# Expert stage of a fused attention and MoE kernel: the second halves of the weight split divided between VectorE and GpSimd and moved to the end of a tile

## Chip, cores, metric

One core of a Trainium2 chip. The metric is device time in microseconds (us) of one execution. TensorE is called PE below, VectorE DVE, ScalarE ACT, GpSimd POOL and SyncE SP, as the profile names them.

## The reference, cut to what matters

Linear attention (8 batches, 8 heads, 576 rows, 64 columns) gives 4608 rows of 512. A gated product with four weight matrices follows, and then the stage that the change touches, a top-1 mixture of 8 experts:

```python
logits = x @ w_gate                       # 4608 x 8
expert_idx = np.argmax(logits, axis=1)
gate_w = probs[np.arange(N), expert_idx]  # softmax of the logits
for e in range(E):
    mask = expert_idx == e
    h = np.maximum(x[mask] @ w1[e], 0.0)  # 512 -> 1024
    out[mask] = gate_w[mask, None] * (h @ w2[e])  # 1024 -> 512
```

## The kernel before

**Precision.** All products are of float32 data in three passes (`split3`, L166): each operand is split into a high part, rounded to the type that PE multiplies (`fp32r`), and a low part, which is the operand less its high part; high by high, high by low and low by high are summed. Every operand of PE so costs a rounding copy (the high part) and a subtraction (the low part).

**Tiles.** The expert stage (from L849 on, in the blocks of `stage2`) works on tiles of 128 rows of one expert. A tile's row numbers stand in a table that the program makes from the counts, and so do the tile's expert and a planned chunk number (below). With the inputs used there are 40 tiles: 5, 4, 5, 1, 5, 5, 8 and 7 for the eight experts. Tiles 0 to 2 are written out, tiles 3 to 38 run in a loop on each engine (`tiles`, one iteration a `tile(g)` or `period(g)`), and the last is written out again.

**One tile on PE** (`tile`, in the PE block): the first product of tile g in two halves (24 matmuls), the transposition of the gathered rows of tile g+1 (4, L1669), and the second product of tile g-1 (24). PE waits in front of them for semaphores that stand for: the rows' low part (`xt_lo`), the rectified halves (`relu_done`), the turned h's low part (`ht_lo`), a result copied out (`y_sb`), and the weights' low part (`w_lo`).

**One tile on the other engines, before.** ACT: four rectifying pieces of the first half times two (8 ACTIVATEs, L1244), the rows' high part (L1200), the high parts of the weight chunks that the table gives this tile (`tile_chunks`, L809), the next gate (L1210), the turned h's high part (L1251). DVE: 8 pieces of the second half (L1451), with the rows' low part (L1428) after the third of them, then the turning of h in 32 by 32 blocks (STREAM_TRANSPOSE, L1461), the copy of the result (L1435), the turned h's low part (L1466). POOL (`period`): gather of tile g+2 by an indirect DMA (L1058, L1061), the low parts of this tile's weight chunks (L1104), scatter of tile g-1 (L1068, L1072).

**Weight chunks.** An expert's weights are 4 chunks of 128 x 2048 (1 MB): two of w1, two of w2. SP loads them into 4 slots (`ahead`), ACT writes the high part into a ring of 8 chunks, then POOL subtracts and writes the low part. SP loads chunk c into its slot when the low part of chunk c-4 is made. The table row CH says up to which chunk a tile goes: it is made on DVE by a chain of small operations (L1541 to L1569) from the tiles' experts, as early as the ring allows and no later than the products need. With these inputs the table of before gives 26 chunks to tiles: two chunks to each of tiles 12, 13 and 15, one to twenty others. Chunks 4 and 5 are written out before the loop.

**The first tiles.** POOL gathers the rows of tiles 1 and 2 (`first_gather`, L1040) when the gate of the tile before is taken over (`gate_set`). For tile 1, ACT copies the gate aside (`gnext`, L1204, which increments `gate_saved`) right after the rows' high part, and takes it over (L1210, `gate_set`) after the rectifying of tile 0.

The loop of chunks, as each engine that has a part in it runs it (L922 to L933):

```python
def tile_chunks(eng, g, body):
    first = table(m, eng, CH, g - 1, CPE, NCH)
    end = table(m, eng, CH, g, CPE, NCH)
    chunks(eng, first, end, body)
```

`table` (L823) is a load of a table entry into a register with a range check.

Of the kernel before, what the change touches and what calls it, by code (L numbers as in the profile page):

```python
# [29 lines left out]
ds = bass.ds  # L30
# [795 lines left out]
def stage2(nc, m, t):  # L826

    with ExitStack() as ctx:
# [25 lines left out]
        w_hi, w_lo = m["w_hi"], m["w_lo"]  # L854
        lg_mm, lg_shift, lg_exp = sem("s2_lg_mm"), sem("s2_lg_shift"), sem("s2_lg_exp")
# [90 lines left out]
        def _(sp):  # L946
# [69 lines left out]
        def _(pool):  # L1016
# [68 lines left out]
            for g in range(1, FIRST):  # L1085
                pool.wait_ge(gate_set, g)
# [36 lines left out]
            last1, last2 = last_of(pool, 1), last_of(pool, 2)  # L1123
            keep_gate(last)
            tile_chunks(pool, last1, weights)
            scatter(last2)
            tile_chunks(pool, last, weights)
# [5 lines left out]
        def _(act):  # L1133
# [93 lines left out]
            def h_high(g):  # L1227
                late = not isinstance(g, int)
                if late:
                    act.wait_ge(w_lo, NCH)  # L1230
                elif g > 0:
                    act.wait_ge(y_mm, g)
# [50 lines left out]
            tile_chunks(act, last, weights)  # L1283
# [3 lines left out]
        def _(dve):  # L1287
# [156 lines left out]
            def relu_moved(g):  # L1444
# [30 lines left out]
            dve.sem_inc(h_turned, 1)  # L1475
            turns(dve, turn)
# [58 lines left out]
            for h in range(2):  # L1535
# [5 lines left out]
            linked(dve.tensor_scalar(ch, ch, 1.0 / CPE, 1.0, ALU.mult, ALU.min), base)  # L1541
            linked(dve.scalar_tensor_tensor(ch, ch, 1.0, ex, ALU.add, ALU.add), base)

            linked(dve.scalar_tensor_tensor(ahead_of[:, 0:last_g], ex[:, 1:last_g + 1], 1.0 / CPE,
                                            ex[:, 2:last_g + 2], ALU.add, ALU.max), base)
            linked(dve.scalar_tensor_tensor(ahead_of[:, 0:last_g], ahead_of[:, 0:last_g], 2.0 / CPE,
                                            ex[:, 3:last_g + 3], ALU.add, ALU.max), base)
            linked(dve.tensor_tensor(ch[:, 0:last_g], ch[:, 0:last_g], ahead_of[:, 0:last_g], ALU.max), base)

            linked(dve.scalar_tensor_tensor(ahead_of[:, 1:last_g], ex[:, 0:last_g - 1], early_w2,  # L1550
                                            ex[:, 2:last_g + 1], ALU.add, ALU.min), base)
            linked(dve.scalar_tensor_tensor(ch[:, 1:last_g], ahead_of[:, 1:last_g], 2.0,
# [252 lines left out]
```

## Time and profile before

| | |
|---|---|
| median of 3 runs | 1511.0 us (1509.08, 1511.07, 1511.0) |
| profiled execution, its own time | 1509.39 us |
| its span in the profile | 1507.7 us |
| PE busy | 1473.6 us, 98% of the span |
| mean granted TensorE clock | 0.993 |
| expert stage | about 1036 to 1498 us of the span |

The span is what the trace covers; the own time of the execution is 1.7 us longer. The profile names a group of instructions by line, engine, operation and tiles (out<-in); most buffers lie in one tile called `arena`, the ring is `big`, the split rows and h are `xs`. PEq, ACTq and so on are an engine's sequencer, which runs register instructions.

### The profile page before, as it was taken

The page shows a single profiled execution, that of the slowest core. Times are in us where ns is not written, and L with a number is a line of the kernel's source. Part 1 is how long each engine was busy: PE and PEld are TensorE (multiplying, and loading weights), DVE is VectorE, ACT ScalarE, POOL GpSimd, SP SyncE. Part 2 cuts the span into 40 slices and gives each one's busy share as a digit, 9 for nine tenths or more (in the row PEclk, how much of TensorE's full clock was granted, in tenths as well). Part 3 has the DMA queues.
Part 4 walks back from the last instruction along what each step waited for, and adds up shares of the span by engine and source line. Part 5 has one row for each costly group of instructions (what it writes and reads, how often), then busy time and mean ns, then how long its engine had stood idle before and what let it go on. Part 6 is the DMA issues. An engine that isn't in the chain of part 4 may idle for free.

```text
span 1507.7 us, 28846 instructions
## 1 busy us (share of the span) xinstructions
PE 1473.6 (98%) x8070; PEld 1274.8 (85%) x8071; DVE 979.4 (65%) x1877; ACT 713.0 (47%) x1512; POOL 630.7 (42%) x681
## 2 busy tenths in 40 slices
PE   7999999999999999999999999999999899999997
PEld 6999999999978888888888888887888778888885
DVE  5688888888825374655637465535677777777663
ACT  5688788788812122121212212143566566656442
POOL 6676676676810021020202102021667776665221
PEclk9999999999999999999999999999999999999999
DMA  7354344344430202021120202134424433321110
GB/s 254 115 142 107 104 107 107 103 108 127 109 122 0 71 15 84 0 84 28 56 70 14 84 0 84 29 131 153 167 96 141 163 116 130 125 73 49 40 48 23
DMA packets 84601, 134.67 MB, mean 89 GB/s; under 512 B 50016, under 2 KB 50272, under 8 KB 80338
## 3 DMA queue, kind: packets, MB, share of 16 engines
q1 hardware_dynamic: 76978, 114.01, 25.2%
q0 software_dynamic: 7584, 20.17, 4.2%
q8 instruction: 21, 0.34, 0.1%
q14 instruction: 18, 0.15, 0.0%
HBM read 104.26 MB, written 30.94 MB: 90 GB/s over the span
## 4 chain that ended last, share of the span: by engine, by line
PE 67%; DVE 1%; DMA 1%; POOL 1%; issue 1%; ACT 1%; POOLq 0%; ACTq 0%; DVEq 0%
PE bank L166 65%; PE bank L1669 1%; POOL big L1104 1%; DVE xs L1466 1%; DMA arena<-rows_scratch,ids 1%; ACT arena L1244 0%; DMA out<-arena,ids 0%; DVE arena L1451 0%; PE bank L1600 0%; PE bank L1705 0%; PE bank L1619 0%; PE bank L1608 0%; ACT big L809 0%; PE bank L1594 0%; DVE xs L1428 0%
## 5 line engine op out<-in xcount | busy, mean ns | idle before, releaser
L166 PE MATMUL bank<-big,xs 128*128 (+1 forms) x2088 | 492.6, 395 | 14.7 <-DVE big L609 8.1
L166 PEld LDWEIGHTS bank<-big,xs 128*128 128x128 f32 x2088 | 391.7, 189 | 96.7 <-issue 15.8
L166 PE MATMUL bank<-xs,big 128*128 128x512 f32 x1728 | 397.4, 391 | 2.7 <-PEq L215 2.7
L166 PEld LDWEIGHTS bank<-xs,big 128*128 128x128 f32 x1728 | 324.7, 188 | 70.3 <-issue 2.9
L166 PE MATMUL bank<-big 128*128 128x512 f32 (+1 forms) x1632 | 325.8, 348 | 2.0 <-POOL big L305 1.4
L166 PEld LDWEIGHTS bank<-big 128*128 128x128 f32 (+1 forms) x1632 | 255.8, 165 | 36.2 <-POOL big L305 1.7
L1021 POOL TENSOR_TENSOR arena<-arena 128x512 f32<-128x512 f32 x32 | 39.8, 1255 | 440.5 <-DMA arena<-rec_scratch 440.2
L1397 DVE TENSOR_TENSOR arena<-arena,bank 128x512 f32<-128x512 f32 x72 | 49.4, 686 | 246.0 <-PE bank L166 246.0
L1157 ACT COPY arena<-bank 128x512 f32<-128x512 f32 x72 | 42.3, 587 | 306.9 <-PE bank L166 302.6
L1322 DVE CUSTOM_DVE_ANT_0 arena<-arena 128x512 f32<-128x512 f32 x256 | 159.5, 688 | 14.9 <-ACT arena L1177 14.7
L1451 DVE TENSOR_SCALAR arena<-bank,gate 32x256 f32<-32x256 f32 x288 | 138.9, 482 | 44.5 <-PE bank L166 40.1
L703 PE MATMUL bank<-arena 128*128 128x66 f32 (+1 forms) x1152 | 147.6, 269 | 0.0
L1244 ACT ACTIVATE arena<-bank,gate 32x256 f32<-32x256 f32 x288 | 134.6, 467 | 17.0 <-PE bank L166 13.9
L703 PEld LDWEIGHTS bank<-arena 128*128 128x128 f32 x1152 | 142.3, 191 | 0.2
L1104 POOL TENSOR_TENSOR big<-arena,big (+1 forms) x28 | 131.9, 4716 | 21.6 <-ACT big L809 10.3
L180 POOL TENSOR_TENSOR kqs<-kqraw,kqs 128x256 fp32r<-128x256 f32 (+1 forms) x160 | 130.1, 813 | 12.8
L507 ACT ACTIVATE arena<-arena 128x256 f32<-128x256 f32 (+1 forms) x320 | 110.3, 399 | 50.0 <-DVE arena L633 40.0
L166 PE MATMUL bank<-wphis,kqs 128*128 128x256 f32 x864 | 130.9, 291 | 0.3
L621 DVE TENSOR_REDUCE absmax<-bank 128x4 f32<-128x512 f32 (+1 forms) x160 | 100.7, 629 | 23.3 <-PE bank L166 22.6
L633 DVE TENSOR_TENSOR arena<-bank,absmax 128x512 f32<-128x512 f32 (+1 forms) x160 | 102.2, 639 | 18.4 <-ACT arena L507 0.5
L166 PEld LDWEIGHTS bank<-wphis,kqs 128*128 128x128 f32 x864 | 111.3, 189 | 1.7 <-DVE arena L633 1.2
L305 POOL TENSOR_TENSOR big<-qeraw,big 128x768 fp32r<-128x768 f32 x32 | 58.7, 1836 | 88.8 <-DMA kqraw<-kq 79.3
(175 smaller groups left out, 1395.0 us busy)
## 6 DMA issues: line engine op xcount, KB each, us to landing
arena<-we SPq DMA_DIRECT2D x32, 1024.0 KB, 4.8
kqraw<-kq SPq DMA_DIRECT2D x32, 576.0 KB, 3.8
rows_scratch<-arena SPq DMA_DIRECT2D x36, 256.5 KB
xT_scratch<-arena SPq DMA_DIRECT2D x32, 288.0 KB
arena<-v SPq DMA_DIRECT2D x64, 128.0 KB, 2.4
arena<-xT_scratch SPq DMA_DIRECT2D x8, 1024.0 KB, 5.4
arena<-rec_scratch SPq DMA_DIRECT2D x64, 128.0 KB, 3.8
arena<-w3T SPq DMA_DIRECT2D x8, 512.0 KB, 3.4
```

Of the source, the lines that this page charges most:

```text
L166: ins = nc.tensor.matmul(out, left[a], right[b], start=first and n == 0, stop=last and n == 2)
L180: pool.tensor_tensor(m["kqs"][:, 1, u, cols], m["kqraw"][:, u, cols], m["kqs"][:, 0, u, cols].bitcast(F32), ALU.subtract).then_inc(m["kq_l ...
L305: eng.tensor_tensor(qes[:, 1, :, cols], qeraw[:, :, cols], qes[:, 0, :, cols].bitcast(F32), ALU.subtract).then_inc(qlo_done[n], 1)
L507: last = act.activation(ke[:, rows[0]:rows[-1] + 1, s * P:(s + 1) * P], pm[:, rows[0]:rows[-1] + 1, 0], ACT.Exp, scale=1.0 - 2.0 * s)
L621: dve.tensor_reduce(absmax[:, bank, 0:n], proj_ps[bank][:, 0:2 * n * P].rearrange("p (t a f) -> p t a f", t=n, a=2), AX.X, ALU.max, apply_ ...
L633: dve.tensor_tensor(pm[:, rows[0]:rows[-1] + 1], proj_ps[bank][:, 0:2 * n * P].rearrange("p (t a f) -> p t a f", t=n, a=2), absmax[:, bank ...
L703: last = pe.matmul(kv_ps[:, s, cols[0]:cols[1]], ke[:, r, s * P:(s + 1) * P], v[:, u, slots[0]:slots[1]].rearrange("p t d -> p (t d)"), st ...
L1104: pool.tensor_tensor(ring[:, 1, ds(at, CW)], ahead[:, ds(slot, CW)], ring[:, 0, ds(at, CW)].bitcast(F32), ALU.subtract).then_inc(w_lo, 1)
L1244: last = act.activation(hq[a * Q:(a + 1) * Q, b * QF:(b + 1) * QF], h_ps[0][b * Q:(b + 1) * Q, a * QF:(a + 1) * QF], ACT.Relu, scale=m["ga ...
L1322: dve.tensor_tensor_reduce(products[e % 2], x2[:, q, 0:DM], m["wgrows"][:, e * DM:(e + 1) * DM], 1.0, 0.0, ALU.mult, ALU.add, lg[:, n:n + ...
L1397: dve.tensor_tensor(abf[:, j % 2], asb[:, j % 2], b_ps[j % 2][:], ALU.mult).then_inc(ab_f, 1)
L1451: last = dve.tensor_scalar(hq[a * Q:(a + 1) * Q, b * QF:(b + 1) * QF], h_ps[1][b * Q:(b + 1) * Q, (a - 2) * QF:(a - 1) * QF], m["gate"][b ...
```

## The change

The low part of a chunk is made in halves: DVE subtracts the first 1024 columns, POOL the other 1024 (for chunks 4 and 5, before the loop, POOL still makes all 2048). A semaphore `w_lo2` counts DVE's halves, and everything that waited for `w_lo` (SP's loads, PE's products, ACT at the end) waits for both.

On ACT the chunks' high parts move from behind the rows' high part to the end of the tile, behind the turned h's high part. On DVE the halves stand at the end of the tile, behind the turned h's low part, and the rows' low part stands behind all eight pieces and ahead of the turning. On POOL the order becomes scatter of tile g-2, chunks of tile g-1, gather of tile g+2. The gather of tile 2's rows waits for `gate_saved` in place of `gate_set`. The table is made by another chain, two operations longer, with one more addition for the end; for these inputs it gives two chunks to tiles 13 and 14 and one to each of 22 others between 3 and 28 (none to 19 and 24).

```diff
@@ SP
                 for u in range(SLOTS):
                     sp.wait_ge(w_lo, SLOTS * i + u - SLOTS + 1)
+                    sp.wait_ge(w_lo2, SLOTS * i + u - SLOTS + 1)
                     load(SLOTS * i + u, u)
@@ POOL
             for g in range(1, FIRST):
-                pool.wait_ge(gate_set, g)
+                pool.wait_ge(gate_set if g == 1 else gate_saved, g)
                 pool.wait_ge(xtr_mm, g)
                 first_gather(g)
...
-            def weights(c):
-                at, slot = ((c % RING) * CW, (c % SLOTS) * CW) if isinstance(c, int) else (
-                    pool.snap((c % RING) * CW), pool.snap((c % SLOTS) * CW))
+            def weights(c, n=HW):
+                at, slot = ((c % RING) * CW + CW - n, (c % SLOTS) * CW + CW - n) if isinstance(c, int) else (
+                    pool.snap((c % RING) * CW + CW - n), pool.snap((c % SLOTS) * CW + CW - n))
                 pool.wait_ge(w_hi, c + 1)
-                pool.tensor_tensor(ring[:, 1, ds(at, CW)], ahead[:, ds(slot, CW)],
-                                   ring[:, 0, ds(at, CW)].bitcast(F32), ALU.subtract).then_inc(w_lo, 1)
+                pool.tensor_tensor(ring[:, 1, ds(at, n)], ahead[:, ds(slot, n)],
+                                   ring[:, 0, ds(at, n)].bitcast(F32), ALU.subtract).then_inc(w_lo, 1)
...
-            weights(CPE)
+            weights(CPE, CW)
             gather(FIRST + 1)
-            weights(CPE + 1)
-            scatter(1)
+            weights(CPE + 1, CW)
 
             def period(g):
+                scatter(g - 2)
+                tile_chunks(pool, g - 1, weights)
                 gather(g + 2)
-                tile_chunks(pool, g, weights)
-                scatter(g - 1)
@@ ACT
             def tile(g):
                 relu_moved(g)
                 rows_high(g + 1, False)
-                tile_chunks(act, g, weights)
                 next_gate(g + 1)
                 turned_h_high(g)
+                tile_chunks(act, g, weights)
@@ DVE
-                for n, (a, b) in enumerate(quarters(2, 2)):
-                    if n == 3:
-                        rows_low(g + 1)
+                for a, b in quarters(2, 2):
...
             def tile(g):
                 relu_moved(g)
+                rows_low(g + 1)
                 turn_h(g)
                 result(g - 1)
                 turned_h_low(g)
+                tile_chunks(dve, g, weights)
+
+            def weights(c):
+                at, slot = dve.snap((c % RING) * CW), dve.snap((c % SLOTS) * CW)
+                dve.wait_ge(w_hi, c + 1)
+                dve.tensor_tensor(ring[:, 1, ds(at, HW)], ahead[:, ds(slot, HW)],
+                                  ring[:, 0, ds(at, HW)].bitcast(F32), ALU.subtract).then_inc(w_lo2, 1)
@@ PE, in front of each use of a chunk in both products
                         pe.wait_ge(w_lo, CPE * e + c * FF // CW + 1)
+                        pe.wait_ge(w_lo2, CPE * e + c * FF // CW + 1)
```

## Rows read from the trace of the kernel before

**Rows 1.** The page, busy time of each engine, here PE's.
```profile
PE 1473.6 (98%) x8070; PEld 1274.8 (85%) x8071; DVE 979.4 (65%) x1877; ACT 713.0 (47%) x1512; POOL 630.7 (42%) x681
```

**Rows 2.** Waits of PE from 900 us on: who waited for whom, total us, times, longest.
```profile
PE bank L166 <- DVE xs L1466: 5.8, 2, 3.9
```

**Rows 3.** All instructions of line 1466 (turned h's low part): ns min/median/max.
```profile
L1466 DVE TENSOR_TENSOR xs<-hturn,xs x36: 1224/1826/5608, 1073.0 to 1481.8; 128x1024 fp32r<-128x1024 f32 x36
```

**Rows 4.** Timeline, 1178 to 1250 us: start us, us, instructions, [idle before <-releaser].
```profile
1188.38 10.01 POOL L1104 TENSOR_TENSOR big<-arena,big  x2 [1.16 <-issue]
1188.67 5.32 DVE L1466 TENSOR_TENSOR xs<-hturn,xs 128x1024 fp32r<-128x1024 f32 x1
...
1194.19 13.87 PE L166 MATMUL bank<-big,xs 128*128 x48 [3.86 <-DVE xs L1466]
...
1234.48 11.18 PE L166 MATMUL bank<-big,xs 128*128 x48 [1.96 <-DVE xs L1466]
```

**Rows 5.** Busy time by stretch, 1190 to 1200 us; PEclk is the granted clock.
```profile
1190.00:1200.00 10.00, 6.14 (x17) 4.65 (x16) 8.54 (x10) 1.21 (x3) 9.04 (x4) 0.66 0.31 107
```

**Rows 6.** Timeline, 1036 to 1125 us: one tile with one chunk and no stall.
```profile
1100.78 1.91 ACT L809 CAST big<-arena  x1 [0.44 <-issue]
...
1103.10 4.63 POOL L1104 TENSOR_TENSOR big<-arena,big  x1 [1.22 <-ACT big L809]
...
1104.56 1.25 DVE L1461 STREAM_TRANSPOSE hturn<-arena 128x1024 f32<-128x1024 f32 x1 [0.97 <-PE bank L166]
...
1105.89 1.05 ACT L1251 CAST xs<-hturn 128x1024 fp32r<-128x1024 f32 x1 [2.04 <-DVE hturn L1461]
...
1109.91 1.47 DVE L1451 TENSOR_SCALAR arena<-bank,gate 32x256 f32<-32x256 f32 x3 [1.11 <-PE bank L166]
1110.07 11.17 PE L166 MATMUL bank<-big,xs 128*128 x48
...
1111.73 0.69 DVE L1428 TENSOR_TENSOR xs<-bank,xs 128x512 fp32r<-128x512 f32 x1 [0.35 <-ACT xs L1200]
...
1112.45 2.48 DVE L1451 TENSOR_SCALAR arena<-bank,gate 32x256 f32<-32x256 f32 x5
...
1115.93 1.25 DVE L1461 STREAM_TRANSPOSE hturn<-arena 128x1024 f32<-128x1024 f32 x1 [1.00 <-PE bank L166]
```

**Rows 7.** Timeline of PE: the rows' transposition that ends two first products, nine tiles apart.
```profile
1177.89 0.60 PE L1669 MATMUL bank<-ident,arena 128*128 128x128 f32 x4
...
1291.32 0.60 PE L1669 MATMUL bank<-ident,arena 128*128 128x128 f32 x4
```

**Rows 8.** Timeline, 1018 to 1046 us: the gather of tile 2's rows and PE.
```profile
1025.27 0.19 ACT L1204 COPY gnext<-arena 128x1 f32<-128x1 f32 x1
...
1028.93 0.96 POOL L1040 DMA_INDIRECT arena<-rows_scratch,ids  x1 [11.06 <-ACT gate L1210]
...
1036.84 0.66 PE L1669 MATMUL bank<-ident,arena 128*128 128x128 f32 x4 [2.28 <-DMA arena<-rows_scratch,ids]
```

**Rows 9.** Chain of waits, 1164 to 1174 us: ACT's sequencer at its first table load.
```profile
1167.26 0.05 ACTq L823
```

**Rows 10.** Timeline, 1145 to 1180 us: a tile of two chunks on ACT.
```profile
1168.96 3.72 ACT L809 CAST big<-arena  x2 [0.43 <-issue]
```

**Rows 11.** Line 1061, the gathers in the loop: from issue to landing.
```profile
DMA to landing us min/median/max: 3.3/3.4/4.6
```

**Rows 12.** Timeline, 1036 to 1125 us: DVE at the end of the table's chain.
```profile
1053.62 0.69 DVE L1428 TENSOR_TENSOR xs<-bank,xs 128x512 fp32r<-128x512 f32 x1 [1.68 <-ACT xs L1200]
```

**Rows 13.** Timeline of the attention stage: two subtractions between SBUF operands, started near each other, twice.
```profile
192.11 1.54 POOL L180 TENSOR_TENSOR kqs<-kqraw,kqs 128x256 fp32r<-128x256 f32 x1
192.11 0.95 DVE L305 TENSOR_TENSOR big<-qeraw,big 128x768 fp32r<-128x768 f32 x1
...
225.71 0.74 POOL L180 TENSOR_TENSOR kqs<-kqraw,kqs 128x256 fp32r<-128x256 f32 x1
225.74 1.53 DVE L305 TENSOR_TENSOR big<-qeraw,big 128x768 fp32r<-128x768 f32 x1
```

More of the change, by code:

```diff
@@ L854, in stage2 @@
         w_hi, w_lo = m["w_hi"], m["w_lo"]
+        w_lo2 = sem("s3_w_lo2")
+        HW = CW // 2
         lg_mm, lg_shift, lg_exp = sem("s2_lg_mm"), sem("s2_lg_shift"), sem("s2_lg_exp")
@@ L1111, in _ @@
             pool.wait_ge(tabs, 2)
-            weights(CPE)
+            weights(CPE, CW)
             gather(FIRST + 1)
-            weights(CPE + 1)
-            scatter(1)
+            weights(CPE + 1, CW)
             def period(g):
+                scatter(g - 2)
+                tile_chunks(pool, g - 1, weights)
                 gather(g + 2)
-                tile_chunks(pool, g, weights)
-                scatter(g - 1)
             last = tiles(pool, period, 2)
-            last1, last2 = last_of(pool, 1), last_of(pool, 2)
+            last1, last2, last3 = (last_of(pool, k) for k in (1, 2, 3))
+            scatter(last3)
+            tile_chunks(pool, last2, weights)
             keep_gate(last)
+            scatter(last2)
             tile_chunks(pool, last1, weights)
-            scatter(last2)
-            tile_chunks(pool, last, weights)
             scatter(last1)
@@ L1230, in h_high @@
                     act.wait_ge(w_lo, NCH)
+                    act.wait_ge(w_lo2, NCH)
                 elif g > 0:
@@ L1282, in _ @@
             relu(last)
-            tile_chunks(act, last, weights)
             h_high(last)
@@ L1473, in tile @@
                 turned_h_low(g)
+                tile_chunks(dve, g, weights)
[4 more added lines that the diff above has]
+                                  ring[:, 0, ds(at, HW)].bitcast(F32), ALU.subtract).then_inc(w_lo2, 1)
             dve.sem_inc(h_turned, 1)
+            dve.sem_inc(w_lo2, CPE + 2)
             turns(dve, turn)
@@ L1539, in _ @@
             early_w2 = W1C / CPE
[L1541 to L1552, printed above, removed]
+            one, two = slice(1, last_g + 1), slice(2, last_g + 2)
+            most = slice(0, last_g)
+            linked(dve.tensor_scalar(ch, ch, 1.0 / CPE, 1.0 / CPE, ALU.mult, ALU.add), base)
@@ new lines, in _ @@
+            linked(dve.scalar_tensor_tensor(ch, ch, 1.0, ex, ALU.min, ALU.add), base)
+            linked(dve.tensor_scalar_add(ch, ch, 1.0), base)
+            linked(dve.scalar_tensor_tensor(ahead_of[:, most], ex[:, one], early_w2, ex[:, two], ALU.add, ALU.max), base)
+            linked(dve.scalar_tensor_tensor(ch[:, most], ahead_of[:, most], early_w2, ch[:, most], ALU.add, ALU.max), base)
+            linked(dve.scalar_tensor_tensor(ahead_of[:, most], ex[:, most], early_w2, ex[:, one], ALU.add, ALU.min), base)
@@ L1553, in _ @@
+            linked(dve.scalar_tensor_tensor(ch[:, most], ahead_of[:, most], 2.0, ch[:, most], ALU.add, ALU.min), base)
+            linked(dve.scalar_tensor_tensor(ch[:, 1:last_g], ahead_of[:, 0:last_g - 1], 2.0 + 2.0 / CPE,
                                             ch[:, 1:last_g], ALU.add, ALU.min), base)
-            linked(dve.scalar_tensor_tensor(ch[:, 2:last_g], ahead_of[:, 1:last_g - 1], 2.0 + 2.0 / CPE,
-                                            ch[:, 2:last_g], ALU.add, ALU.min), base)
@@ L1557, in _ @@
-            linked(dve.scalar_tensor_tensor(ch[:, 0:last_g], ex[:, 1:last_g + 1], early_w2,
-                                            ch[:, 0:last_g], ALU.add, ALU.max), base)
+            linked(dve.tensor_scalar_min(ch[:, FIRST:FIRST + 1], ch[:, FIRST:FIRST + 1], (CPE + FIRST) / CPE), base)
+            linked(dve.scalar_tensor_tensor(ahead_of[:, most], ex[:, most], early_w2, ex[:, one], ALU.add, ALU.max), base)
+            linked(dve.scalar_tensor_tensor(ch[:, most], ahead_of[:, most], early_w2, ch[:, most], ALU.add, ALU.max), base)
@@ L1559, in _ @@
             linked(dve.tensor_scalar(ch, ch, float(CPE), float(NCH), ALU.mult, ALU.min), base)
             linked(dve.tensor_scalar_min(tabf[:, 0], tabf[:, 0], float(E - 1)), base)
-            linked(dve.memset(tabf[:, 2, FIRST - 1:FIRST], float(CPE + FIRST - 1)), base)
+            linked(dve.memset(tabf[:, 2, FIRST - 2:FIRST], float(CPE + FIRST - 1)), base)
             linked(dve.tensor_copy(tabf[:, 3], ends[:, E - 1:E].to_broadcast([P, GMAX])), base)
@@ L1567, in _ @@
             linked(dve.tensor_scalar_add(tabf[:, 3, 3:4], tabf[:, 3, 0:1], -3.0), base)
+            linked(dve.tensor_scalar_add(tabf[:, 3, 4:5], tabf[:, 3, 0:1], -4.0), base)
             dve.tensor_copy(m["tab"][:, 0:ROW], m["tabf"][:, 0:ROW]).then_inc(tabs, 1)
@@ L1692, in second_product @@
                         pe.wait_ge(w_lo, CPE * e + W1C + j * DM // CW + 1)
+                        pe.wait_ge(w_lo2, CPE * e + W1C + j * DM // CW + 1)
                     if j % DC == 0:
```

## The prediction

> **What bounds the kernel now.** First the page: PE is busy for 98% of the span [rows 1], so a change here can win only what PE loses by waiting, and can lose more. Next the waits of PE in the second part of the run: nearly all is the turned h's low part (L1466), twice, 5.8 us [rows 2]. The timeline shows why. At 1188.67 DVE starts L1466, alone 1.22 us [rows 3], while POOL has been in a chunk's subtraction since 1188.38; it takes 5.32 us, as it ends only about a microsecond after POOL's instruction of 4.6 us. PE waits 3.86 us. The same happens at 1228.6 and costs 1.96 us [rows 4]. After the long wait the granted clock of 1190 to 1200 us is 0.66, that is, part of it at 1.2 GHz [rows 5], and the 48 matmuls take 13.87 us in place of 11.17; after the short one they take 11.18 [rows 4, 6]. All that is lost there is read from two transpositions nine tiles apart: 1291.32 - 1177.89 = 113.43 us [rows 7]; a tile without a stall takes 1115.93 - 1104.56 = 11.37 [rows 6], nine of them 102.3. So 11.1 us are lost around the expert with one tile, where three tiles have two chunks. One more loss lies at the stage's start: PE waits 2.28 us for the gather of tile 2's rows [rows 8].
>
> **Part 1: the stalls of before go (-11.1 us).** L1466 no longer meets a POOL subtraction: POOL's half of a chunk starts when the high part is there, behind L1466. The planned chunks also end a tile or more ahead of their use. What is late next is part 3.
>
> **Part 2: the early gather (-2.3 us).** Gather 2 is issued at 1028.93 and lands by 1036.8, 7.9 us. With `gate_saved` it may follow L1204, which ends at 1025.46: issue at about 1025.7. Even with 7.9 us it lands at 1033.6, and PE asks for it at 1036.84 - 2.28 = 1034.56 [rows 8]. All 2.28 us go. What follows on PE moves along; the loads of chunk 4 and 5 don't, but ACT casts them beside PE's work.
>
> **Part 3: the new chain at a tile's end, one chunk.** I follow it from the start of the turning (L1461), t = 0, with the rows of a tile without a stall.
> - ACT's turned high part starts at 1105.89 - 1104.56 = 1.33 [rows 6]. Then ACT's sequencer must load two table entries and compute addresses. In before this began at 1167.26, ahead of the rows' high part, and the cast started at 1168.96, 1.70 later [rows 9, 10]. Now it begins when L1251 is issued: cast from 3.04 to 4.95 (1.91 long).
> - DVE's half: between the end of the cast and POOL's start behind it are 1103.10 - 1102.69 = 0.41 us [rows 6]. DVE's own lag has no row; it is bounded by 0.1 (L1466 behind L1251, without registers) and 0.5. I take 0.41, since its steps are the same. The half is 128x1024 between SBUF operands, as L1466: 1.22 [rows 3]. It ends at 6.6.
> - The next tile's eight pieces: 1.47 + 2.48 [rows 6], to 10.6; the rows' low part 0.69, to 11.3; PE's first matmul 0.20 behind it (1193.99 to 1194.19 in [rows 4]), and 0.05 for the added wait: 11.5.
> - PE has room for 11.37 - 0.3 = 11.06: the turning starts 0.3 us after PE began the next first product (1110.07 + half of 11.17, and 1115.93 [rows 6]).
>
> So PE stalls 0.45 us. But after a stall the turning, which had waited for PE's second product, starts 0.2 us ahead of PE's next first product in place of 0.3 behind it; the next tile's chain has 0.5 us more room and gives no stall. The 22 tiles with one chunk come in runs of 10, 4, 4 and 4, every other one stalls: 11 x 0.45 = **+5.0 us**. With a lag between 0.1 and 0.5 this is 1.5 to 6.5.
>
> **Part 4: two tiles with two chunks.** The second cast ends at 3.04 + 3.72 = 6.76 [rows 10], but POOL's first half, which waited for DVE's first, has the port from 6.6 for 4.63 / 2 = 2.3 us, to 8.8. DVE's second half then ends about 1.1 later (as L1466 did), at 9.9, and PE starts at 9.9 + 4.65 + 0.25 = 14.8: a stall of 3.7. The next tile, also with two, starts 0.5 ahead: 3.2. Together **+7.0 us**. Bounds: 4 if DVE's second half comes ahead of POOL's first, 11 if both of POOL's halves come ahead.
>
> **Part 5: the clock.** A stall of 3.86 was followed by slow matmuls, 2.7 us, one of 1.96 was not [rows 4]. Stalls of 3.7 and 3.2 lie between: 0 to 5.4 us for the two. I take one, **+2.7**.
>
> **Edits costed at nothing.** ACT's next pieces start at t = 5.0 (or 6.8) and its rows' high part is done by 9.5 (or 11.3), before DVE asks (10.6, 13.9). The rows' low part moved behind five pieces: in place of them before, the idle 1.0 us ahead of the turning stays. POOL's scatter DMA waits for the result copy at t = 2, then issues; its half waits for the port until 6.6 and ends at 8.8; then the gather's two small copies and its DMA, issued at about t = 11. It lands 3.3 to 4.6 later [rows 11], and PE asks for it at t = 16.5. SP waits longer for a free slot (POOL ends at 8.8, before at 1107.73 - 1104.56 = 3.2), but a chunk is loaded four chunks ahead. The added waits of PE run ahead of its matmuls. The table's three extra small operations lie where DVE waited 1.68 us for ACT [rows 12]. The tail is as before.
>
> **Sum.** 1509.4 - 11.1 - 2.3 + 5.0 + 7.0 + 2.7 = 1510.7; without a clock loss 1508.0, with two 1513.4. The profiled execution (1509.39) is 1.6 us faster than the median of the three runs (1511.0), which may hold more clock loss, in before as in the change. I say **1510.5 us**, no difference beyond 0.2% (3 us, about what a measurement of this kernel can tell from no change).
>
> **Rivals.**
> 1. *POOL gets to the port first* in every tile with a chunk. Both engines are released by the same cast, and what counts is who starts first: with both at 192.11, DVE ran unhindered in 0.95 and POOL took 1.54; with POOL at 225.71, 0.03 ahead, POOL took 0.74 and DVE 1.53 [rows 13]. The Trainium skill, SBUF — State Buffer, section SBUF: two separate sides, says of the pair of ports shared by VectorE and GpSimd that the instruction that starts first holds it to its end and the other blocks; by that rule, and the trace agrees, an order off by some hundredths decides here. DVE's half then ends at 5.36 + 2.3 + 1.1 = 8.75 in place of 6.6, the turning of the next tile waits for DVE too, and each of 22 tiles takes 11.37 + 2.1: +46, the double ones +11, with -13.4: 1553 us. Against it: POOL's addresses need an addition more each, and its instructions start later behind a register step than the others'. It decides from a lead of about 0.02 us of POOL on. Chance 0.12.
> 2. *The chain is shorter than I think*, or DVE's second half slips in ahead of POOL's first: parts 3 to 5 cost 1.5 + 4 + 0 to 2.7; 1502 to 1504 us, faster. For it: the lag of DVE is my largest guess, and each stall has a neighbour that absorbs it. Against it: ACT's 1.7 us of registers are measured. Chance 0.25.
> 3. *The chain is longer by 0.2 us and both double tiles lose the clock*: 6.5 + 8 + 5.4, 1516 us, slower. For it: the sequencer work of DVE (two table loads behind L1466) isn't in the trace and I assumed that it ends before the cast does. Chance 0.15.
> 4. *The new order doesn't take effect*, as the stalls move to other waits of the same size: within my forecast.
>
> **Chances.** Forecast 0.48, of it some at either edge; faster 0.28, within 0.2% 0.42, slower 0.30. The forecast's own range is 1507 to 1514. The range is 1502 to 1518: it takes in rivals 2 and 3 and leaves out rival 1 and a little on either side.
>
> **What would show it.** The intervals between L1669 in tiles 4 to 13 alternate between 11.37 and about 11.8. Two of 14 to 15 us stand at tiles 14 and 15, the expert's single tile no longer has one of 18. L1466 takes 1.22 us in all 36 tiles. DVE's half takes 1.22 when it is first and about 3.4 as the second of two; POOL's takes 2.3, and 3.4 where it waited. If POOL's halves take 2.3 everywhere and DVE's 3.4, rival 1 holds. If PE has no idle before L166 in tiles with one chunk, part 3 was too dear. If PE still waits before the third transposition of the stage, part 2 fails.

## The result and the profile after

The changed kernel takes 1513.4 us (median of 20 executions, 1510.15 to 1516.1); the kernel before, run beside it, 1510.65 us (20 executions). The ratio is 1.0020, with a 95% interval of 1.0011 to 1.0029: slower by 0.2%, where I had said 1510.5 and no difference. The profiled execution took 1513.48 us (before: 1509.39), with a span of 1511.4.

First the page's busy times, then the waits of PE from 900 us on (who waited for whom, total us, times, longest); they answer to [rows 1, 2]:

```profile
PE 1475.7 (98%) x8070; PEld 1274.1 (84%) x8071; DVE 984.6 (65%) x1907; ACT 710.8 (47%) x1512; POOL 596.6 (39%) x681
```

```profile
PE bank L166 <- DVE xs L1431: 10.4, 13, 3.8
```

PE waits for one thing only, the rows' low part (now L1431), 13 times: the 11 tiles and the two double ones that parts 3 and 4 name. The turned h's low part has gone from the list, and its line shows why (before, [rows 3], the median was 1826 ns):

```profile
L1467 DVE TENSOR_TENSOR xs<-hturn,xs x36: 1224/1226/1228, 1072.0 to 1485.6; 128x1024 fp32r<-128x1024 f32 x36
```

**Early gather.** The timeline at the stage's start, as [rows 8]: the gather is issued 1.62 us behind the second transposition (before: 1028.93 - 1024.12 = 4.81), and the third transposition has no wait. The second transposition before, then the rows after:

```profile
1024.12 0.63 PE L1669 MATMUL bank<-ident,arena 128*128 128x128 f32 x4
```

```profile
1025.61 0.63 PE L1679 MATMUL bank<-ident,arena 128*128 128x128 f32 x4
...
1027.23 0.96 POOL L1043 DMA_INDIRECT arena<-rows_scratch,ids  x1 [7.87 <-ACT gnext L1207]
...
1035.90 0.60 PE L1679 MATMUL bank<-ident,arena 128*128 128x128 f32 x4
```

The interval between the two transpositions is 10.29 us; before it was 1036.84 - 1024.12 = 12.72. The gain is 2.43.

**The chain of a tile with one chunk.** Timeline, 1060 to 1094 us: two tiles after each other, the first with a stall, the second without.

```profile
1069.50 1.25 DVE L1462 STREAM_TRANSPOSE hturn<-arena 128x1024 f32<-128x1024 f32 x1 [1.34 <-issue]
...
1070.83 1.05 ACT L1255 CAST xs<-hturn 128x1024 fp32r<-128x1024 f32 x1 [3.13 <-DVE hturn L1462]
1071.99 1.22 DVE L1467 TENSOR_TENSOR xs<-hturn,xs 128x1024 fp32r<-128x1024 f32 x1 [0.67 <-ACT xs L1255]
...
1072.61 1.91 ACT L809 CAST big<-arena  x1 [0.73 <-issue]
...
1074.95 1.23 DVE L1481 TENSOR_TENSOR big<-arena,big  x1 [1.74 <-ACT big L809]
...
1075.04 3.39 POOL L1107 TENSOR_TENSOR big<-arena,big  x1 [0.93 <-ACT big L809]
1076.20 3.96 DVE L1452 TENSOR_SCALAR arena<-bank,gate 32x256 f32<-32x256 f32 x8
...
1080.19 0.69 DVE L1431 TENSOR_TENSOR xs<-bank,xs 128x512 fp32r<-128x512 f32 x1
...
1080.85 1.25 DVE L1462 STREAM_TRANSPOSE hturn<-arena 128x1024 f32<-128x1024 f32 x1
...
1081.29 5.74 PE L166 MATMUL bank<-big,xs 128*128 x24 [0.58 <-DVE xs L1431]
...
1086.22 1.22 DVE L1481 TENSOR_TENSOR big<-arena,big  x1 [1.66 <-ACT big L809]
1086.29 3.41 POOL L1107 TENSOR_TENSOR big<-arena,big  x1 [0.84 <-ACT big L809]
```

From the turning (t = 0 at 1069.50) the cast runs from 3.11 to 5.02, DVE's half from 5.45 to 6.68, the pieces to 10.66, the rows' low part to 11.38, and PE starts at 11.79. With the prediction's 11.06 of room that is a stall of 0.73, and the next turning starts 0.44 us ahead of PE, so that the tile after it has none. (By its interval, 12.24, the tile loses 0.87; the missing 0.14 is taken up in the part on the prediction.) From turning to turning DVE takes 1080.85 - 1069.50 = 11.35, just under PE's 11.37: so the chain makes PE wait when it starts behind PE, and doesn't when it starts ahead. The intervals between L1679 show the pattern: 12.24, 11.36, 12.15, 11.41, 12.10, 11.38 and so on. (The wait that the profile prints, 0.58, is shorter than what the tile loses, since the matmuls before a pause are shown to their own end.) DVE starts its half 0.06 to 0.09 us ahead of POOL, in every first chunk; POOL's subtraction then takes 3.4 us, DVE's 1.22.

**The two double tiles.** Timeline, 1180 to 1236 us, to be held against [rows 4]:

```profile
1192.50 1.23 DVE L1481 TENSOR_TENSOR big<-arena,big  x1 [1.64 <-ACT big L809]
1192.57 6.73 POOL L1107 TENSOR_TENSOR big<-arena,big  x2 [0.81 <-ACT big L809]
...
1194.29 2.77 DVE L1481 TENSOR_TENSOR big<-arena,big  x1 [0.56 <-ACT big L809]
...
1202.17 7.26 PE L166 MATMUL bank<-big,xs 128*128 x24 [3.78 <-DVE xs L1431]
...
1216.70 5.72 PE L166 MATMUL bank<-big,xs 128*128 x24 [1.35 <-DVE xs L1431]
```

The stretch around the first of these stalls, as [rows 5]:

```profile
1200.00:1210.00 10.00, 7.83 (x30) 6.35 (x31) 7.06 (x9) 6.47 (x8) 6.12 (x5) 0.83 0.45 154
```

After the stall of 3.78 the clock is down (0.83 as a mean of the stretch, so part of it at 1.2 GHz), and 24 matmuls take 7.26 in place of 5.72. The second stall is only 1.35, and from one first product to the next are 1216.70 - 1202.17 = 14.53 us, as many as between the two tiles' first halves on DVE (1192.50 and 1207.03).

**The account.** I count what the stage loses by its last 36 transpositions. These are their first and last rows, after and then before:

```profile
1063.27 0.60 PE L1679 MATMUL bank<-ident,arena 128*128 128x128 f32 x4
...
1476.88 0.60 PE L1679 MATMUL bank<-ident,arena 128*128 128x128 f32 x4
```

```profile
1064.26 0.60 PE L1669 MATMUL bank<-ident,arena 128*128 128x128 f32 x4
...
1473.13 0.60 PE L1669 MATMUL bank<-ident,arena 128*128 128x128 f32 x4
```

A tile without a stall takes 11.365 (eight at the end of the stage take 90.9), 35 of them 397.8. After, 413.6 less 397.8 is **15.8 us lost**; before, 408.9 less 397.8, **11.1**. Of the 15.8, 8.4 are the 11 single stalls, 7.2 the two double tiles with their clock (intervals of 16.95 and 12.99), 0.2 the rest. So the stage lost 4.7 more and the gather gave 2.4 back: +2.3, against +2.75 between the medians. The profiled executions stand 4.1 apart: the one of after was already 1.5 us late at the second transposition (1025.61 against 1024.12), before any part of the change, and the last 0.4 lie outside the span. Over all the kept traces that transposition starts between 1024.12 and 1027.53, and the trace of before is the earliest of them; so part of the scatter between executions arises ahead of the stage.

### The profile page after: what moved, and what is told of

The parts are those of the page before. It is cut to its first block and busy times, and to the rows that moved or that the text cites. A ratio compares the mean times of both kernels' runs of the same rounds, so it can differ in the third digit from the quotient of the medians.

```text
span 1511.4 us, 29641 instructions
## 1 busy us (share of the span) xinstructions
PE 1475.7 (98%) x8070; PEld 1274.1 (84%) x8071; DVE 984.6 (65%) x1907; ACT 710.8 (47%) x1512; POOL 596.6 (39%) x681
## 5 line engine op out<-in xcount | busy, mean ns | idle before, releaser
L166 PE MATMUL bank<-big,xs 128*128 (+1 forms) x2088 | 495.5, 395 | 18.6 <-DVE xs L1431 10.4
L1248 ACT ACTIVATE arena<-bank,gate 32x256 f32<-32x256 f32 x288 | 134.3, 466 | 14.6 <-PE bank L166 11.5
L180 POOL TENSOR_TENSOR kqs<-kqraw,kqs 128x256 fp32r<-128x256 f32 (+1 forms) x160 | 126.6, 791 | 12.8
L1075 POOL DMA_INDIRECT out<-arena,ids x38 | 69.3, 1824 | 118.1 <-DVE arena L1438 117.1
L1107 POOL TENSOR_TENSOR big<-arena,big (+1 forms) x28 | 97.8, 3495 | 24.0 <-ACT big L809 19.6
```

Source lines behind the costliest of these rows:

```text
L166: ins = nc.tensor.matmul(out, left[a], right[b], start=first and n == 0, stop=last and n == 2)
L180: pool.tensor_tensor(m["kqs"][:, 1, u, cols], m["kqraw"][:, u, cols], m["kqs"][:, 0, u, cols].bitcast(F32), ALU.subtract).then_inc(m["kq_l ...
L1075: pool.indirect_dma_start(t["out"], bass.IndirectOffsetOnAxis(ids[:, 0:1], 0), src, None, bounds_check=N - 1, oob_is_err=False).then_inc(s ...
L1107: pool.tensor_tensor(ring[:, 1, ds(at, n)], ahead[:, ds(slot, n)], ring[:, 0, ds(at, n)].bitcast(F32), ALU.subtract).then_inc(w_lo, 1)
L1248: last = act.activation(hq[a * Q:(a + 1) * Q, b * QF:(b + 1) * QF], h_ps[0][b * Q:(b + 1) * Q, a * QF:(a + 1) * QF], ACT.Relu, scale=m["ga ...
```

## The experiments

The loss of the loop, in the table at the end, is counted as above. Lines shift by a few from kernel to kernel.

**The early gather alone, and the change without it.**

```diff
@@ e1: the kernel before, POOL
-                pool.wait_ge(gate_set, g)
+                pool.wait_ge(gate_set if g == 1 else gate_saved, g)
@@ e2: the changed kernel, POOL: the same line the other way
```

> The kernel before with one edit of the change alone: the gather of tile 2's rows waits for gate_saved. Theory (this is a gain of 2.4 us that the rest of the change hides): about 1508.2 us, 0.9984 of before, and the interval between the second and third transposition of the stage 10.3 us in place of 12.7; the stall around the one-tile expert stays. Rival (the gather's landing is set by other DMA traffic, and the shorter interval in the changed kernel came from elsewhere): no change.

> The changed kernel with that one edit undone (gate_set again). Theory: 2.4 us slower than the changed kernel, about 1515.8 us, 1.0035 of before, so that the rest of the change alone loses about 5 us. Rival: as the changed kernel, 1513.4 us.

e1: 1507.11 us, 0.9976 of before (0.9967 to 0.9985). e2: 1514.32, 1.0027 (1.0016 to 1.0038), so 0.9 us slower than the whole change. In the traces the interval is 10.29 with the early gather and 12.64 without it, 2.35 apart. Both results allow that figure, and only e1's shows a gain by itself: its interval is -5.0 to -2.3 us, while those of e2 and of the change overlap widely, so that the times of these two don't tell 2.4 us from nothing. In e2's profiled execution the clock fell behind the wait for the gather, which before, in the execution of [rows 8], it didn't; the same stretch in e2, then before:

```profile
1041.00:1045.00 4.00, 4.00 (x14) 3.13 (x14) 0.69 (x1) 0.59 (x3) 0.00 (x0) 0.59 0.94 348
```

```profile
1041.00:1045.00 4.00, 4.00 (x20) 3.27 (x19) 2.67 (x8) 1.92 (x1) 0.05 (x1) 1.00 1.02 430
```

The 16.64 us that follow the third transposition in e2 are 14.91 in the change. A wait of 2.2 us can so cost 2.4 or 4.1. How often it costs the more wasn't settled.

**The rows' low part at other places of DVE's order.**

```diff
@@ the changed kernel, DVE: relu_moved; e3 with 6, e5 with 3
-                for a, b in quarters(2, 2):
+                for n, (a, b) in enumerate(quarters(2, 2)):
+                    if n == 6:
+                        rows_low(g + 1)
@@ tile
-                rows_low(g + 1)
```

> The changed kernel with VectorE's rows' low part after the sixth of the eight pieces. Theory (PE's stalls in tiles with one chunk are the end of a chain: cast, VectorE's half, eight pieces, rows' low part, PE): the rows' low part ends 1.0 us earlier, 0.7 us were missing, so the 11 stalls of 0.76 us go, and the two long ones shrink by about 1 us each: 8.4 + 2 = 10 us faster than the changed kernel, about 1503 us, 0.995 of before. Rival (PE is held by the port contention or by the added waits on w_lo2, wherever the rows' low part stands): stalls stay, 1513 us. Second rival (the turning then starts late and takes the stall over): the intervals stay at 11.75 on average.

> The changed kernel with VectorE's rows' low part back after the third piece, as before the change. Theory (chain): the pieces now start at t = 6.7 behind VectorE's half, the third ends at 8.1, but ScalarE's rows' high part ends only at 9.5, since its own pieces wait for the cast's end at 5.0; VectorE idles 1.3 us in the middle and its loop takes 12.7 us in place of 11.37. With some 0.6 us of slack at the start of each run of tiles, 22 tiles lose about 1.3 us each and the double ones 3: 30 us of stalls in place of 15.8, about 1528 us, 1.011 of before. So this part of the change was needed by the other. Rival (the place of the rows' low part is of no weight, VectorE has idle time in every tile): 1513 us.

e3: 1504.8 us, 0.9959 (0.9944 to 0.9974). e5: 1530.08, 1.0136 (1.0114 to 1.0159). Waits of PE in e3, then in e5:

```profile
PE bank L166 <- DVE xs L1431: 6.2, 2, 3.1
```

```profile
PE bank L166 <- DVE xs L1431: 15.6, 21, 0.8
PE bank L166 <- POOL big L1107: 4.4, 2, 2.9
```

In e3 every one-chunk tile takes 11.36 to 11.40; the two pieces taken out from ahead of the rows' low part (0.99 us) are more than the 0.73 by which the chain was too long. Its two double tiles lose 8.4 us (intervals 14.73 and 16.37), 1.2 more than in the change: both waits of PE are 3.08 us, the first is followed by 24 matmuls in 5.74 us (granted clock 1.00 from 1196 to 1202), the second by 24 in 7.37 (0.77 from 1210 to 1216), and no stall comes behind it to take the lost clock back. So the length of the wait alone doesn't tell whether the clock falls. In e5 the rows' low part comes too early for ACT, whose rows' high part is behind the cast and eight pieces. The timeline of e5, one tile:

```profile
1069.34 1.25 DVE L1464 STREAM_TRANSPOSE hturn<-arena 128x1024 f32<-128x1024 f32 x1 [1.00 <-PE bank L166]
...
1078.11 0.59 ACT L1203 CAST xs<-bank 128x512 fp32r<-128x512 f32 x1
1078.73 0.69 DVE L1431 TENSOR_TENSOR xs<-bank,xs 128x512 fp32r<-128x512 f32 x1 [1.23 <-ACT xs L1203]
...
1082.04 1.25 DVE L1464 STREAM_TRANSPOSE hturn<-arena 128x1024 f32<-128x1024 f32 x1
```

DVE idles 1.23 us with five pieces queued behind it, each of which the turning needs. From turning to turning it takes 1082.04 - 1069.34 = 12.70, above PE's 11.37, and so nearly every tile with a chunk stalls, by 1.2 to 1.3. The place that fits is a window, behind ACT's high part and ahead of PE's need: behind all eight pieces the subtraction costs 8.6 us more than in e3, behind three 25.3 more.

**The share of each engine.**

```diff
@@ the changed kernel: e6 (DVE 512 columns) and e7 (DVE 1536)
-        HW = CW // 2
+        HW, VW = CW - 512, 512
...
+                dve.tensor_tensor(ring[:, 1, ds(at, VW)], ahead[:, ds(slot, VW)],
```

> The changed kernel with VectorE making 512 of a chunk's 2048 columns and GpSimd 1536. Theory (chain): VectorE's part is 0.53 us shorter, the stall of every other tile falls from 0.76 to about 0.2 us; a double tile keeps its stall, since GpSimd's first part is as much longer: about 6 us faster than the changed kernel, 1507.5 us, 0.998 of before. Rival (the port: GpSimd holds it for 3.4 us a chunk in place of 2.2 and so blocks VectorE more): as the changed kernel or slower.

> The changed kernel with VectorE making 1536 columns and GpSimd 512. Theory (chain, with a tile after a stall 0.74 us ahead): the part is 0.53 us longer, stalls of about 0.5 and 0.75 us take turns in place of 0 and 0.75, 22 us in all in place of 15.2: about 6.8 us slower than the changed kernel, 1520 us, 1.006 of before. Rival (the port, of which VectorE and GpSimd together now hold less): faster than the changed kernel.

e6: 1508.4 us, 0.9984 (0.9972 to 0.9996). e7: 1519.25, 1.0060 (1.0037 to 1.0083). DVE's part took 693 ns and 1759 ns in place of 1225. In e6 each single stall shrank by what DVE's part did, from 12.15 - 11.37 = 0.78 to 0.27 (11.64). In e7 the chain from turning to turning went above 11.37 (1082.58 - 1070.74 = 11.84), and every tile with a chunk stalls, by 0.92 and 0.37 in turn (12.29, 11.74). DVE's half is on the path to PE; POOL's, up to 4.0 us long in e6, has no wait of PE in either; in a tile with two chunks it still holds up DVE's second part.

**The halves exchanged: POOL first.**

```diff
@@ e8: the changed kernel; POOL takes columns 0 to 1023, DVE the others
-                    pool.snap((c % RING) * CW + CW - n), pool.snap((c % SLOTS) * CW + CW - n))
+                    pool.snap((c % RING) * CW), pool.snap((c % SLOTS) * CW))
...
-                at, slot = dve.snap((c % RING) * CW), dve.snap((c % SLOTS) * CW)
+                at, slot = dve.snap((c % RING) * CW + HW), dve.snap((c % SLOTS) * CW + HW)
```

> The changed kernel with the halves exchanged: GpSimd makes the first 1024 columns, VectorE the last. The work is the same; the addition of 1024 to both addresses moves from GpSimd to VectorE. In the changed kernel VectorE starts 0.393 us behind the cast's end and GpSimd 0.461, so VectorE has the port first by 0.07 us in all but the second chunks. Theory (who starts first holds the port): GpSimd then starts at 0.40, VectorE at 0.43 to 0.47; GpSimd's half runs in 2.3 us, VectorE's takes 3.4, each tile with a chunk loses 2.15 us, the double ones 5.4: 60 us of stalls in place of 15, about 1558 us, 1.031 of before. Rival (the port is given to VectorE when both ask at about the same time, or the lead is larger than the additions): 1513 us.

1560.83 us, 1.0340 (1.0313 to 1.0368). The same work; one address addition has changed engines. The timeline of e8, one tile, and its waits of PE:

```profile
1085.55 1.91 ACT L809 CAST big<-arena  x1 [0.68 <-issue]
1087.87 2.39 POOL L1107 TENSOR_TENSOR big<-arena,big  x1 [0.77 <-ACT big L809]
1087.96 3.38 DVE L1481 TENSOR_TENSOR big<-arena,big  x1 [1.75 <-ACT big L809]
```

```profile
PE bank L166 <- DVE xs L1431: 43.9, 19, 5.6
```

POOL starts at 1087.87, 0.09 us ahead, and its half takes 2.39; DVE's takes 3.38, although it does what took 1.22. This is the prediction's rival 1: it gave +2.1 us per one-chunk tile, and the intervals are 13.43 and 13.46 against 11.37. In all it gave 57 us for the loop and 1553 for the kernel; the loop lost 63.1, some of it to the clock (granted 0.94 from 1265 to 1345 us, where tiles take up to 15.99). The changed kernel stands 0.07 us on the good side of it.

**PE's wait for the rows read last.**

```diff
@@ e9: the changed kernel, PE: first_product
-                pe.wait_ge(xt_lo, g + 1)
...
                         pe.wait_ge(w_lo2, CPE * e + c * FF // CW + 1)
+                    if c == 0:
+                        pe.wait_ge(xt_lo, g + 1)
```

> The changed kernel, with TensorE's wait for the rows' low part (xt_lo) read last, behind the waits for the relu of the tile before and for both halves of the chunk. Theory: of the 0.41 us between the end of the rows' low part and the first product, about 0.2 are the three waits that TensorE still reads after it, so the first product starts about 0.2 behind it, the single stalls go from 0.76 to about 0.55, those of the two double tiles fall by 0.2 each, together about 2.5 us: 1511, 1.0003 of the kernel before. Rival: the 0.41 us are the way of the signal and the place of the wait has no weight: 1513.4, as the changed kernel.

1510.27 us, 0.9999 (0.9988 to 1.0009), loop loss 13.5. The timeline of e9:

```profile
1080.66 0.69 DVE L1431 TENSOR_TENSOR xs<-bank,xs 128x512 fp32r<-128x512 f32 x1
...
1081.55 4.62 PE L166 MATMUL bank<-big,xs 128*128 x19 [0.38 <-DVE xs L1431]
```

PE now starts 0.20 us behind the rows' low part (before this edit 0.41), and the stalls are 11.92 - 11.37 = 0.55. So half of the 0.41 were the three waits that PE reads after the one that ends last, though their semaphores had long been set.

**The halves in the old order.** e4 is the kernel before with two things of the change, the halves (DVE's at the tile's end, with `w_lo2`) and the early gather. The table, ACT's cast behind the rows' high part, POOL's order and the rows' low part after the third piece are as before (the edit below leaves out the lines of the table's chain and of the last tiles).

```diff
@@ e4 against the changed kernel
 POOL
             def period(g):
-                scatter(g - 2)
-                tile_chunks(pool, g - 1, weights)
                 gather(g + 2)
+                tile_chunks(pool, g, weights)
+                scatter(g - 1)
 ACT
                 rows_high(g + 1, False)
+                tile_chunks(act, g, weights)
                 next_gate(g + 1)
                 turned_h_high(g)
-                tile_chunks(act, g, weights)
 DVE
-                for a, b in quarters(2, 2):
+                for n, (a, b) in enumerate(quarters(2, 2)):
+                    if n == 3:
+                        rows_low(g + 1)
...
-                rows_low(g + 1)
```

> The halves without the new order: the kernel before with its own table, ScalarE's and GpSimd's order, rows' low part after three pieces, with VectorE's half at the end of the tile, GpSimd's half where the whole was, and the early gather. Theory (the order on ScalarE is what makes VectorE's half late; the halves themselves are worth the 11.1 us of the old stalls): VectorE's half no longer waits for the cast and ends before its next pieces are needed, no stall in any tile with one chunk, at most 1 us around the one-tile expert: 1510.65 - 11.1 - 2.4 + 1 = 1498 us, 0.992 of before. Rival (the halves on two engines that share a port cost about as much as the stalls that they remove, in any order): 1506 to 1513 us.

**1497.71 us, 0.9913 (0.9896 to 0.9929)**: faster than both kernels. Its timeline, and its only wait of PE from 900 us on:

```profile
1074.58 1.25 DVE L1483 TENSOR_TENSOR big<-arena,big  x1 [0.91 <-issue]
...
1077.53 1.91 ACT L809 CAST big<-arena  x1 [0.44 <-issue]
...
1079.92 2.41 POOL L1107 TENSOR_TENSOR big<-arena,big  x1 [1.20 <-ACT big L809]
...
1081.31 1.25 DVE L1465 STREAM_TRANSPOSE hturn<-arena 128x1024 f32<-128x1024 f32 x1 [0.76 <-PE bank L166]
```

```profile
PE bank L166 <- DVE big L1483: 0.5, 1, 0.5
```

The cast is made early in the tile, POOL's half follows it at once and is done in 2.4 us, before DVE wants the port; DVE's half follows at the tile's end, with no wait for ACT. The two halves never meet, and DVE waits 0.76 us for PE ahead of the turning: there is room. POOL's halves still meet the turned h's low part (now L1470) in three places at the double tiles, but shorter as they are they hold it up less than in [rows 4]:

```profile
1182.83 4.77 POOL L1107 TENSOR_TENSOR big<-arena,big  x2 [0.77 <-issue]
...
1186.46 2.23 DVE L1470 TENSOR_TENSOR xs<-hturn,xs 128x1024 fp32r<-128x1024 f32 x1 [0.45 <-ACT xs L1255]
```

L1470 takes 2.23 us there, the longest of the three, in place of the 5.32 of before, and PE doesn't wait for it. Of the 11.1 us that the loop of before lost, 10.4 are gone.

**Which part of the new order costs.** Two kernels from e4.

```diff
@@ e10 against e4: ACT, then DVE
-                tile_chunks(act, g, weights)
                 next_gate(g + 1)
                 turned_h_high(g)
+                tile_chunks(act, g, weights)
...
-                    if n == 3:
+                    if n == 6:
                         rows_low(g + 1)
@@ e11c against e4: DVE
-                    if n == 3:
-                        rows_low(g + 1)
...
                 relu_moved(g)
+                rows_low(g + 1)
                 turn_h(g)
```

> The halves in the old order of the queues (1497.7 us), with one difference: ScalarE casts the chunk at the tile's end, as in the changed kernel, and the rows' low part follows the sixth of VectorE's pieces. Theory: it is the place of the cast, at the tile's end, that puts a chain of 11 us between the turning and the next tile's first product, so one-chunk tiles stall little (the chain there was 0.3 us inside its room with the rows' low part after the sixth piece) and tiles with two chunks stall 3 us each, perhaps with a loss of clock: 1503 to 1507. Rival: the place of the cast has no weight, the order of VectorE's pieces alone made the loss: 1498.

> The halves in the old order of the queues (1497.7 us), with one difference: VectorE makes its eight pieces first and then the rows' low part, as in the changed kernel. Theory: the order of VectorE's work costs only where its half of the chunk waits for a cast at the tile's end; with the cast made early, VectorE still waits 0.8 us for TensorE ahead of the turning, the rows' low part ends a microsecond later and long before TensorE needs it: 1498, no stall on the rows' low part. Rival: the place of the rows' low part costs by itself, as its move from eight to six pieces gained 8.6 us in the changed kernel: 1503 to 1507, with waits of TensorE for it.

e11c: 1499.64 us, 0.9937 (0.9922 to 0.9952), loop loss 3.1 against 0.7. The order of DVE's pieces alone costs about 2 us (with five executions of each, and intervals that overlap a little); 2.6 of the 3.1 are in three intervals among the double tiles (12.45, 11.74, 12.48), next to nothing in the one-chunk tiles. With the cast early the rival's 5 to 9 us are not there; the theory said none at all, and one wait of PE for the rows' low part, of 0.8, is there.

e10: 1519.68 us, 1.0060 (1.0040 to 1.0080), loop loss 25.3: well above the 1503 to 1507 that I expected. The three double tiles lose 3.4, 5.5 and 6.1 us (intervals 14.73, 16.82, 17.51, two with a loss of clock), 15.0 together, where I had allowed 9 to 12. The other 10 lie in the tiles with one chunk or none, and have a cause that I hadn't seen. The timeline of the tile that loses most (interval 13.76):

```profile
1304.76 1.02 POOL L1075 DMA_INDIRECT out<-arena,ids  x1 [0.96 <-POOL ids L1071]
...
1309.56 1.92 ACT L809 CAST big<-arena  x1 [0.94 <-issue]
1309.79 0.69 DVE L1439 COPY arena<-bank 128x512 f32<-128x512 f32 x1 [2.31 <-DMA out<-arena,ids]
1310.40 1.22 DVE L1470 TENSOR_TENSOR xs<-hturn,xs 128x1024 fp32r<-128x1024 f32 x1
...
1311.95 2.39 POOL L1107 TENSOR_TENSOR big<-arena,big  x1 [3.11 <-ACT big L809]
1311.95 3.47 DVE L1483 TENSOR_TENSOR big<-arena,big  x1 [0.34 <-issue]
...
1319.53 2.77 PE L166 MATMUL bank<-big,xs 128*128 x11 [1.99 <-DVE xs L1432]
```

With POOL's old order the scatter stands behind POOL's half, which now waits for a late cast. The scatter lands late, DVE's result copy waits 2.31 us for it, DVE comes to its half so late that it has lost its lead, and POOL holds the port: 3.47 in place of 1.22, and a stall of 1.99. This is the only chunk of e10 in which DVE's half lost the pair of ports; the tile lost 2.4 us of the 10. Another lost 2.1 (interval 13.45; PE waits 0.99 for POOL's half, itself behind the late cast), and the rest is 0.1 to 0.8 in each of a dozen and more, most of which have DVE's result copy wait about 2 us for the scatter. What the trace suggests is that once the cast is late the scatter has to stand ahead of the chunk, as it does in the change; no run has this one difference. The 22 us of e10 over e4 are thus no measure of the cast's place in the changed kernel; that the double tiles' part of them is 15 is read from the trace, and what the change's own table saves of it (two double tiles in place of three) had no run of its own.

The lot, with the loop's loss:

| kernel | us | ratio to before | loop loss |
|---|---|---|---|
| before | 1510.65 | 1 | 11.1 |
| the change | 1513.4 | 1.0020 | 15.8 |
| e1 before, early gather | 1507.11 | 0.9976 | 10.9 |
| e2 change, late gather | 1514.32 | 1.0027 | 15.9 |
| e3 change, rows' low part after six | 1504.8 | 0.9959 | 8.5 |
| e5 change, after three | 1530.08 | 1.0136 | 32.3 |
| e6 change, DVE a quarter | 1508.4 | 0.9984 | 10.2 |
| e7 change, DVE three quarters | 1519.25 | 1.0060 | 22.3 |
| e8 change, POOL first | 1560.83 | 1.0340 | 63.1 |
| e9 change, rows' wait last | 1510.27 | 0.9999 | 13.5 |
| e4 halves, old order | 1497.71 | 0.9913 | 0.7 |
| e11c e4, rows' low part last | 1499.64 | 0.9937 | 3.1 |
| e10 e4, cast at the end | 1519.68 | 1.0060 | 25.3 |

## Why the prediction was right or wrong

**Part 1** holds: L1467 takes 1.22 in all 36 tiles, and the 11.1 us that I read from two transpositions are what the account of the whole loop gives.

**Part 2** holds: 2.43 in the trace for 2.3. The gather is issued at 1027.23, which is the 1025.7 that I said plus the 1.5 us by which this execution is late there.

**Part 3** is the step that failed, by the size of its term (and, for the sign, the last step of the sum, below). The mechanism is as put: a chain from the turning through cast, half, pieces and rows' low part to PE, over its room in every other tile, with a neighbour that absorbs it. But the stall is 0.76, not 0.45, and 11 of them 8.4 us, not 5.0. Unrounded, my chain adds up to 11.47 us; in the tile shown it is 11.79, and 11.71 at the next stall (1093.09 to 1104.80). The largest part of that is the last link, 0.41 and not 0.25: I took 0.20 from a start of PE that reads no wait behind the one that ends last, and added 0.05 for the new wait, where e9 shows that the three waits read behind the rows' one cost 0.2 together. The half ended at 6.68 where I had 6.6, mostly because the cast of this tile starts at 3.11 (about 3.05 in later ones), and small gaps between DVE's instructions, for which I had nothing, make up the rest. The room, too, was nearer 11.00 than 11.06: I halved a group of 48 matmuls that is shown to its last matmul's own end (11.17), where from its first matmul to the transposition behind it are 11.01 (1087.22 to 1098.23). And behind a stall the product takes 5.58 to that transposition (1081.29 to 1086.87) in place of 5.50. At the next stall this gives 11.71 - 11.00 + 0.08 = 0.79, which is what its interval of 12.15 says. Where a chain of 11.5 is held against a room of 11, a tenth of a microsecond is a fifth of the term, times 11. DVE's lag behind the cast, for which I took 0.41 between 0.1 and 0.5, is 0.43 in the tile shown and 0.39 in the next.

**Parts 4 and 5** were right in the first double tile (3.7 forecast, 3.78 measured; DVE's second half, held up by POOL's first, ends 9.9 us after the turning as I said, though it takes 2.77 and not 3.4) and in one loss of clock, and too dear in the second tile: 1.35, not 3.2. The chain of DVE, ACT and POOL runs on at its own pace, 14.53 us from one first product to the next, while PE's matmuls are slow, so the 1.5 us that the clock costs are taken out of the next stall (in e3, where the clock falls behind the second stall, they are not). The two tiles lose 7.2 us in all, about the 7.0 of part 4 alone; part 5's 2.7 were counted on top of a wait that hides them.

**The sum.** By its terms -11.1 - 2.3 + 5.0 + 7.0 + 2.7 = +1.3; measured -11.1 - 2.4 + 8.4 + 7.2 + 0.2 = +2.3. The errors (+3.4 in part 3, -2.5 in parts 4 and 5) nearly cancel, by luck. What took the forecast to the other sign was the last step: the sum said +1.3 over the profiled execution, and that one was 1.6 below the median of the runs shown. Carried over to the median this is 1512.3; I argued that the median might hold more clock loss in both kernels, stayed at 1510.5, and so gave the median of the change a number that belongs to a single execution. With 20 runs the median of before is 1510.65, still 1.3 above its profiled execution.

**The rivals.** Rival 1 didn't come about, by 0.07 us, and e8 shows its price for a tile as worked out (2.1 us), the whole at 1560.8 for 1553; my range left it out with 0.12. Its figure of 0.02 us of lead isn't borne out: in e10 POOL has the ports at equal starts as shown (1311.95), where in [rows 13] DVE had them. Rival 2, the shorter chain, is what e3 makes of it: 1504.8, a little above its 1502 to 1504. Rival 3 was right in that the chain is longer, by 0.3, and wrong in the clock (one loss, not two); the truth lies between it and the forecast. Rival 4 describes the outcome too: stalls of one kind (11.1 us) went and stalls of another (15.8) came. The change is within the range of 1502 to 1518.

What no part of the prediction asked is what the new order is for. I costed halves and order together against before; e4 shows that the halves and the early gather win 13 us, and that the new order (table, late cast, POOL's order, pieces first) gives these back and 3 more. How these 16 us divide among its parts isn't shown, but for the 2 us of the pieces' order in e11c.

## What to carry to other kernels

Where two subtractions share the pair of ports, put them at different times of the tile rather than side by side: e4 gains because one engine's half is done before the other's begins, while a cast placed just ahead of both makes them start together and puts its own length on the chain. When a change bundles a division of work with a new order, try the division in the old order first. And carry a difference worked out from one execution to the median as a difference: add it to the median, don't compare it with the execution's own time.

## What was not expected

- The lead decides, not the length: exchanging which half needs the address addition moved the start of POOL from 0.07 us behind DVE to 0.09 ahead, and the kernel from 1513.4 to 1560.8 us. The Trainium skill, SBUF — State Buffer, section SBUF: two separate sides, has the rule that whoever starts first holds the shared pair of ports to its end; the first chunks of both kernels agree (DVE 1.22 and POOL 3.4 us in the one, 3.38 and 2.4 in the other). Of smaller leads there are single cases: with DVE 0.05 ahead in one tile of e10 (1132.91 and 1132.96) DVE had the ports, 1.23 and 3.44 us; at equal starts as shown either engine did ([rows 13] and e10's 1311.95).
- Waits whose semaphores are long set aren't free when they are read behind the one that ends last: 0.41 us against 0.20 from release to first matmul, about 2.3 us of the loop, for one wait moved behind three others.
- A stalled chain alternates: the excess shows in every other tile, at nearly its full size, because the stall itself gives the next tile its head start. It holds only while the chain's own round (11.35) is shorter than PE's (11.37); in e5 and e7 it is not, and every tile stalls.
